# Causal scores on 64x64 tiles of TensorE: 24 instructions of 64 columns for 16 of 128, with two head pairs' keys exchanged

## What is computed

```python
def _attn_ref(r, k, v, w, u):            # 2 batches, 8 heads, 768 steps, 48 channels
    state = 0
    for t in range(S):
        y[:, :, t] = r_t @ (state + (u * k_t) v_t^T)
        state = w_t[:, None] * state + k_t v_t^T
x = y by token                           # 1536 x 384
g = elu(x @ w_in); x = g @ w_out         # 384 -> 2048 -> 384
p = domain_probs / sum
out = sum over 4 experts e of p[:, e] * (relu(x @ w1[e]) @ w2[e])
```

## Time and profile before

| what | us |
|---|---|
| median of 3 runs | 646.91 (646.85 to 646.93) |
| profiled execution, its own time | 646.69 |
| its span in the profile | 644.9 |
| TensorE busy in the span | 638.4 |
| VectorE busy | 418.6 |
| GpSimd busy | 296.0 |
| ScalarE busy | 237.1 |

### The profile page before, as it was taken

How to read it: one execution, slowest core, us unless ns; L and a number is a source line. 1 busy time by engine, 2 the same in 40 slices (tenths; PEclk the granted TensorE clock), 3 DMA queues, 4 the chain that set the end, 5 groups by cost and what they waited for, 6 DMA issues and landing times.

```text
span 644.9 us, 13796 instructions
## 1 busy us (share of the span) xinstructions
PE 638.4 (99%) x5046; PEld 591.5 (92%) x5046; DVE 418.6 (65%) x786; ACT 237.1 (37%) x557; POOL 296.0 (46%) x370
## 2 busy tenths in 40 slices
PE   8999999999999999999999999999999999999998
PEld 5998999877788888999999999999999999999997
DVE  7889999865357666565655555565656565656564
ACT  4785555655455554222222222222222222222221
POOL 5897424420499999996029900029900018000000
PEclk9999999999999999999999999999999999999999
DMA  8954454300000233000012100013100011001011
GB/s 322 403 193 137 138 183 164 124 11 1 1 2 1 73 98 99 27 1 1 1 50 99 50 1 0 1 49 99 50 1 0 0 50 50 0 1 49 0 50 50
DMA packets 19043, 42.34 MB, mean 66 GB/s; under 512 B 2608, under 2 KB 8752, under 8 KB 18992
## 3 DMA queue, kind: packets, MB, share of 16 engines
q1 hardware_dynamic: 18704, 41.23, 18.6%
q10 hardware_dynamic: 288, 0.39, 0.2%
HBM read 37.16 MB, written 4.46 MB: 65 GB/s over the span
## 4 chain that ended last, share of the span: by engine, by line
PE 90%; DVE 4%; POOL 3%; issue 1%; DMA 0%; ACT 0%; DVEq 0%; POOLq 0%
PE bank L1365 29%; PE bank L1366 29%; PE bank L1367 29%; POOL w_lo L546 3%; PE bank L1199 1%; PE bank L1278 1%; DVE fr L863 1%; PE bank L1290 1%; DVE fr L882 1%; DVE att L921 0%; DMA rkw<-rkw_dram 0%; DVE w_lo L966 0%; DVE bank L996 0%; PE bank L1232 0%; PE bank L1298 0%
## 5 line engine op out<-in xcount | busy, mean ns | idle before, releaser
L1365 PE MATMUL bank<-x_lo,w_hi 128*128 128x256 f32 (+2 forms) x416 | 138.1, 332 | 0.5 <-POOL w_lo L546 0.3
L1366 PE MATMUL bank<-x_hi,w_lo 128*128 128x256 f32 (+2 forms) x416 | 135.2, 325 | 0.0
L1367 PE MATMUL bank<-x_hi,w_hi 128*128 128x256 f32 (+2 forms) x416 | 135.2, 325 | 0.0
L1366 PE MATMUL bank<-w_hi,g_lo 128*128 128x384 f32 x384 | 129.6, 338 | 0.0
L1367 PE MATMUL bank<-w_hi,g_hi 128*128 128x384 f32 x384 | 129.3, 337 | 0.0
L1365 PE MATMUL bank<-w_lo,g_hi 128*128 128x384 f32 x384 | 129.0, 336 | 0.0
L826 ACT ACTIVATE g_hi<-bank 128x512 fp32r<-128x512 f32 x96 | 57.5, 598 | 144.3 <-DVE bank L1052 122.4
L1365 PEld LDWEIGHTS bank<-x_lo,w_hi 128*128 128x128 f32 x416 | 78.2, 188 | 10.4 <-issue 2.5
L1367 PEld LDWEIGHTS bank<-x_hi,w_hi 128*128 128x128 f32 x416 | 78.3, 188 | 7.4
L1366 PEld LDWEIGHTS bank<-x_hi,w_lo 128*128 128x128 f32 x416 | 78.3, 188 | 7.1
L1045 DVE TENSOR_TENSOR u_sum<-p_copy,bank 128x256 f32<-128x256 f32 x56 | 23.6, 421 | 92.1 <-ACT p_copy L750 91.3
(11 more groups left out here) (134 smaller groups left out, 1258.8 us busy)
## 6 DMA issues: line engine op xcount, KB each, us to landing
raw<-w_dram SPq DMA_DIRECT2D x48, 384.0 KB, 3.7
rkw<-rkw_dram SPq DMA_DIRECT2D x10, 772.5 KB, 4.5
tok<-tok_dram SPq DMA_DIRECT2D x10, 576.0 KB, 5.9
k_blocks_dram<-k_blocks SPq DMA_DIRECT2D x8, 256.0 KB, 4.1
kt_sb<-k_blocks_dram SPq DMA_DIRECT2D x32, 64.0 KB, 2.0
out_dram<-acc SPq DMA_DIRECT2D x10, 192.0 KB, 1.9
rkw<-rkw_dram SPq DMA_DIRECT2D x2, 512.0 KB, 4.4
rkw<-rkw_dram SPq DMA_DIRECT2D x2, 260.5 KB, 3.3
```

The lines of the kernel that those rows point to most:

```text
L1365: pe.matmul(out, wh, ml, start=start, stop=False, skip_group_check=shared)
L1366: pe.matmul(out, wl, mh, start=False, stop=False, skip_group_check=shared)
L1367: return pe.matmul(out, wh, mh, start=False, stop=stop, skip_group_check=shared)
```

## The change

Scores of the chunks 2 to 11 are no longer made for the block that is masked altogether (second half of the keys, first half of the queries). The three others are made one by one, 64 keys by 64 queries: 24 instructions of 64 columns in place of 16 of 128. So that each of the four tiles gets six of them, the first two pairs have the halves of their keys exchanged in `att` (partitions 0 to 63 hold the second half of the keys), and a pair with exchanged keys and one without stand side by side in `att` (`place`).

What follows from it: the rows of `tok` must be exchanged for the first four heads, which takes three transfers in place of one, with rows of three pieces of 192 numbers; the turned keys must be exchanged, which takes three transposes in place of one; the diagonal is set in three instructions for two; both copies wait for all three; the mask is there twice, once exchanged, by two more small transfers at the start.

```diff
+        def exchanged(p):
+            return p < PAIRS // 2
+        def place(c, p):
+            return p if c < FIRST else p % 2 * 2 + p // 2
...
         def diagonal_done(c):
-            return 2 * (c + 1 - FIRST)
+            return 3 * (c + 1 - FIRST)
...
-                sp.dma_start(tok[c % DEEP][:, :], tok_d[c]).then_inc(s_tok[c % DEEP], 16)
+                def columns(t, first):
+                    return t.rearrange("p (s n) -> p s n", s=3)[:, :, first:first + DM // 2]
+                here, there = tok[c % DEEP], tok_d[c]
+                sp.dma_start(columns(here[0:HALF, :], 0), columns(there[HALF:CH, :], 0)).then_inc(s_tok[c % DEEP], 16)
+                sp.dma_start(columns(here[HALF:CH, :], 0), columns(there[0:HALF, :], 0)).then_inc(s_tok[c % DEEP], 16)
+                sp.dma_start(columns(here[:, :], DM // 2), columns(there, DM // 2)).then_inc(s_tok[c % DEEP], 16)
...
+            for rows, others in ((slice(0, HALF), slice(HALF, CH)), (slice(HALF, CH), slice(0, HALF))):
+                sp.dma_start(const[rows, 0:P], const_d[others, C_MASK:C_MASK + P]).then_inc(s_exchanged, 16)
...
+                diagonal(0, 0, HALF, HALF)
+                diagonal(0, HALF, HALF, 0)
+                diagonal(1, 0, CH, 0)
...
-                dve.transpose(k_blocks[:, :, :].rearrange("q t (a j) -> q t a j", a=PAIRS),
-                              raw_k(c).rearrange("q (a t i) -> q t a i", a=PAIRS, i=STRIP)).then_inc(s_kb, 1)
+                dve.transpose(turned[:, 0:2, 0:2, :], strips[:, 2:4, 0:2, :]).then_inc(s_kb, 1)
+                dve.transpose(turned[:, 2:4, 0:2, :], strips[:, 0:2, 0:2, :]).then_inc(s_kb, 1)
+                dve.transpose(turned[:, :, 2:4, :], strips[:, :, 2:4, :]).then_inc(s_kb, 1)
...
-                    dve.wait_ge(s_diag, diagonal_done(c) - 1 + o)
-                    dve.copy_predicated(att[:, o, :, :], masks.bitcast(I32), found).then_inc(s_att, 1)
+                    dve.wait_ge(s_diag, diagonal_done(c))
+                    found = banks["x"][o][:, :].rearrange("p (a t) -> p a t", a=PAIRS // 2)
+                    dve.copy_predicated(att[:, o, :, :].rearrange("p (a b) t -> p a (b t)", b=2),
+                                        both_masks.unsqueeze(1).broadcast_to([P, PAIRS // 2, 2 * CH]).bitcast(I32),
+                                        found).then_inc(s_att, 1)
...
-                        for half in range(2):
-                            keys = slice(p * CH + HALF * half, p * CH + HALF * half + HALF)
-                            ins = pe.matmul(banks["x"][o][HALF * half:HALF * half + HALF, cols], k[rows, keys],
-                                            q[rows, cols], start=True, stop=True)
+                def block(p, o, later, first, count):
+                    rows, at = slice(64 * o, 64 * o + D), HALF * (later != exchanged(p))
+                    out = place(c, p) * CH + first
+                    return pe.matmul(banks["x"][o][at:at + HALF, out:out + count],
+                                     k[rows, p * CH + HALF * later:p * CH + HALF * later + HALF],
+                                     q[rows, p * CH + first:p * CH + first + count], start=True, stop=True)
+                for p in range(PAIRS // 2):
+                    for one in (p, p + PAIRS // 2):
+                        for later in range(2):
+                            for o in range(2):
+                                block(one, o, later, HALF, HALF)
+                    for one in (p, p + PAIRS // 2):
+                        for o in range(2):
+                            ins = block(one, o, 0, 0, HALF)
```

More of the change, by code:

```diff
@@ L294, in bass_linear_attention_elu_ffn_dense_experts, with tok_landed @@
         s_dr = sem("s_dr")
-        mask = const[:, C_MASK:C_MASK + P]
-        ident = const[:, C_ID:C_ID + P]
+        both_masks = const[:, 0:2 * P]
+        mask = const[:, P:2 * P]
+        ident = const[:, 2 * P:3 * P]
         def landed(eng, sems, c):
             eng.wait_ge(sems[c % DEEP], 16 * (c // DEEP + 1))
+        def tok_landed(eng, c):
+            parts = 3 * (c // DEEP + 1) - (2 if c % DEEP < FIRST else 0)
+            eng.wait_ge(s_tok[c % DEEP], 16 * parts)
+        def exchanged(p):
+            return p < PAIRS // 2
+        def place(c, p):
+            return p if c < FIRST else p % 2 * 2 + p // 2
         def raw_q(c):
@@ L532, in bonus_diagonal, with diagonal @@
                 pool.wait_ge(s_py, c)
[L533 to L537, removed]
+                heads = bonus_sb[:, c % 2, :]
+                found = att[:, :, :, :].rearrange("p o a t -> p (o a) t")
+                def diagonal(b, first, count, base):
+                    values = heads[:, b * PAIRS:(b + 1) * PAIRS].unsqueeze(2).broadcast_to([P, PAIRS, count])
+                    pool.affine_select(found[:, b:H:2, first:first + count], values, pattern=[[0, PAIRS], [1, count]],
+                                       compare_op=ALU.is_equal, fill=0.0, base=base, channel_multiplier=-1).then_inc(s_diag, 1)
+                diagonal(0, 0, HALF, HALF)
+                diagonal(0, HALF, HALF, 0)
+                diagonal(1, 0, CH, 0)
             def lo_w(n, half):
@@ L699, in copy_odd @@
             def copy_odd(c):
[L700 removed]
+                tok_landed(act, c)
                 need(act, s_py, c - 1)
@@ L910, in mask_scores @@
                     dve.wait_ge(s_px, c + 1)
+                    if c == FIRST:
+                        dve.wait_ge(s_exchanged, 32)
                     if c < FIRST:
@@ L1189, in scores @@
                 q, k = q_of(c), k_of(c)
[L1190 to L1194, removed]
-                            ins = pe.matmul(banks["x"][o][:, cols], k[rows, cols], q[rows, cols], start=True, stop=True)
-                            continue
-                        for half in range(2):
-                            keys = slice(p * CH + HALF * half, p * CH + HALF * half + HALF)
-                            ins = pe.matmul(banks["x"][o][HALF * half:HALF * half + HALF, cols], k[rows, keys],
-                                            q[rows, cols], start=True, stop=True)
+                if c < FIRST:
+                    for p in range(PAIRS):
+                        cols = slice(p * CH, (p + 1) * CH)
+                        for o in range(2):
+                            rows = slice(64 * o, 64 * o + D)
+                            ins = pe.matmul(banks["x"][o][:, cols], k[rows, cols], q[rows, cols], start=True, stop=True)
+                    ins.then_inc(s_px, 1)
+                    return
+                def block(p, o, later, first, count):
[10 more added lines that the diff above has]
+                    for one in (p, p + PAIRS // 2):
+                        for o in range(2):
+                            ins = block(one, o, 0, 0, HALF)
                 ins.then_inc(s_px, 1)
@@ L1289, in values_even @@
                     columns = STRIP // 2 if b % 3 == 1 else STRIP
-                    pe.matmul(strip_of(yt, b)[0:columns], v[:, first:first + columns], att[:, 0, p, :],
+                    pe.matmul(strip_of(yt, b)[0:columns], v[:, first:first + columns], att[:, 0, place(c, p), :],
                               start=False, stop=True, skip_group_check=True)
             def odd_strip(c, yt, b):
-                return pe.matmul(strip_of(yt, b), v_of(c)[:, b * STRIP:(b + 1) * STRIP], att[:, 1, b // 3, :],
+                return pe.matmul(strip_of(yt, b), v_of(c)[:, b * STRIP:(b + 1) * STRIP], att[:, 1, place(c, b // 3), :],
                                  start=False, stop=True, skip_group_check=True)
             def odd_end(c, yt, b):
-                return pe.matmul(strip_of(yt, b), v_odd[:, c % 2, b // 3, :], att[:, 1, b // 3, :],
+                return pe.matmul(strip_of(yt, b), v_odd[:, c % 2, b // 3, :], att[:, 1, place(c, b // 3), :],
                                  start=False, stop=True, skip_group_check=True)
```

28 lines of the change are left out of this document (16 added, 12 removed).

## The result

The changed kernel takes 649.57 us (median, 649.25 to 650.77), the kernel before 646.92 beside it. The ratio is 1.0045, 95% interval 1.0034 to 1.0055. The change costs 2.65 us, and the measured time lies above the range of the prediction.

What follows compares the result with a forecast made beforehand. TensorE, busy 638.4 of 644.9 us, was taken as the bound, with VectorE pacing chunks 5 to 7. Scores and VectorE gave -0.64, the keys' stall +0.2, about -0.4: 646.5 us, no change; range 645.3 to 648.3.

Steps and rivals of the forecast that it cites:

- Covered work: Diagonal's third instruction hidden by 1.8 us of cover; mask and longer tok transfers at the start costed at nothing.
- The turned keys: Keys' way through memory: tok 0.3 us longer (0 to 0.45), keys 0.6 later, TensorE 0.13 later.
- A stall of about 0.2 us in chunk 6, none elsewhere: TensorE's update waiting for the turned keys: 0.2 us in chunk 6 only, added to the sum.
- the 0.3 us that the prediction had named as a sign that it was wrong: Prediction wrong if an update row stands over 0.3 us behind the row ahead of it.
- rival 3: Turned keys come too late behind tok's short rows; update waits in chunks 3 to 7: 648.8 us, chance 0.13.
- The scores' gain of 0.17 us a chunk: TensorE's score group: 0.70 us for 0.87, 12 turns at 0.058; 1.7 us over ten chunks if TensorE never waits.
- Rival 4: Score MATMULs of 64 columns keep 0.0268 us start to start: 0.43 more a chunk, 651 us, chance 0.06.
- The transposes' 0.13 each: VectorE's three transposes take 0.755 us for 0.63: 0.13 more for each of chunks 2 to 9; bounds zero and 0.36.
- GpSimd's third instruction: Third instruction for the diagonal: some 0.1 us more, hidden by 1.8 us of cover before the copies.
- VectorE sets the pace around chunks 5 to 7: Between chunks 5 and 7 VectorE, at 0.13 us more a chunk, paces TensorE's scores for three chunks.
- The walk: Chunk-by-chunk lateness of TensorE against VectorE's scaled queries: chunk 7's scores 0.21 us late, 0.04 after them.
- chunks 8 to 11 keep all: VectorE has room from chunk 8 on, so four chunks keep 0.17 us each: 0.04 - 4 x 0.17 = -0.64.

Runs made afterwards that it cites:

- a_tok_host: Changed kernel with tok laid out exchanged in memory, so one transfer with rows of 4608 B again; mask transfers stay: 647.22 us, ratio 1.0005.
- b_tok_short: Kernel before with only tok cut into three transfers with rows of 768 bytes, nothing exchanged: 650.90 us, ratio 1.0068.
- a_host_turn_one: a_both_host with one transposition in place of three, leaving out the exchange of the keys that the update reads: 646.69 us, ratio 0.9998 to the kernel before.
- a_both_host: Changed kernel with tok exchanged in memory and both masks in the first transfer of constants: 647.42 us, ratio 1.0007 to the kernel before.
- a_slices_first: Changed kernel with weight slices 10 to 15 issued ahead of chunk 3's tok and the masks: 649.74 us, ratio 1.0042 to the kernel before.

## Why the prediction was wrong

**The step that failed** is the end of *Covered work*: "The two mask transfers and the longer `tok` transfers at the start lie in queues that are filled with weights used later. I cost them at nothing." The weights are used later, but not late enough. The DMA engines have no idle time from 16 to 32 us (a share of 1.02 and more in every window), so work put in makes all behind it late by its full length, and ScalarE reached for the first of the slices 10 to 15 while it was still in the queue. So the term for `tok` at the start, put at nothing, is 1.3 us of queue time for each of two transfers, and the short rows in all cost 2.4 us of the kernel's time. The masks cost about nothing, as was said. a_tok_host and b_tok_short show it from both sides.

**A size that was off**, in *The turned keys*: 0.3 us more for each `tok`, with 0.45 as the upper bound. By the packets above each `tok` took 1.3 us more. I had taken the price per KB from other transfers, with rows of 512 bytes, in a window with the DMA engines a third busy, so the bound was no bound. The load explains only a part: after 40 us, where the queues are emptier, `tok`'s packets still take 51 ns in the mean.

For short rows the Trainium skill (DMA: Bandwidth & Descriptors, section Why small descriptors are slow (HBM only)) gives a fixed 3 cycles a packet beside one for each 32 bytes. By that a row of 768 bytes takes 27 cycles for 24, an eighth more, and one of 4608 bytes 147 for 144: as an estimate 0.2 us on `tok`'s 1.7. The traces disagree: a mixture with such rows lost 19% of the rate (1303 for 1618), and a `tok` transfer took 1.3 us more. The measurement decides.

**The rest of the chain.** "A stall of about 0.2 us in chunk 6, none elsewhere": chunk 6's update did not wait, those of chunks 2, 4 and 5 did, two of them by more than the 0.3 us that the prediction had named as a sign that it was wrong. So rival 3 named the right mechanism (keys that come late behind `tok`), which I gave 0.13; its place, the chunks 3 to 7, was right for the smaller part only. The larger part hit at and before chunk 2, first through the weight slices, which no rival named. The prediction knew the queues to be filled there and put no price on it. That rival 3's 648.8 us lies near the measured time is in part luck.

**What held.** The scores' gain of 0.17 us a chunk: 0.86 for 1.03, with 12 turns of 0.058. Rival 4, a floor of 0.0268 for each MATMUL, is out: it would have shown a row of 1.4, and the row is 0.93. The turns are read from single starts: 107 ns for the first, 58 to 59 for the others. The transposes' 0.13 each: 0.75 for 0.63. GpSimd's third instruction, put at some 0.1 and covered: chunk 6's diagonal takes 1.37 us for 1.22. That VectorE sets the pace around chunks 5 to 7 as soon as the scores are shorter: a_host_turn_one.

**What was off beyond `tok`.** With the transfers undone (a_both_host) 647.4 us stand against the 646.5 of the forecast, so the `tok` step alone does not make the forecast right. The walk had chunk 7's scores 0.21 late; in a_both_host they begin at 97.99, 0.83 late, with chunk 5's late keys (0.4, below) among it. From there on "chunks 8 to 11 keep all" was to give 0.68 by the scores of chunk 11 (those of chunks 7 to 10) and gave 0.16: they begin at 157.40, against 156.73 before. a_both_host's waits name the reason:

```profile
PEld bank L1406 <- DVE x_lo L1034: 0.9, 2, 0.7
...
PEld bank L1406 <- DVE x_lo L1039: 0.4, 1, 0.4
```

One of the two waits for L1034 lies at 118.8 us, where the next tile of x begins: VectorE has room on the average of a slice there, but not at the step that TensorE waits for. In the kernel before, TensorE's operand load has no such wait between 110 and 125 us.

## What to carry to other kernels

A queue that is busy without a gap gives no cover by itself: price added transfer work at its full length, for whatever lies behind it, and look how much slack the first user of that has. Read the price of a row's length in a loaded window, and prefer to rearrange data in memory once over cutting a transfer into short rows. A gain on the busiest engine arrives only in those stretches where no other engine sets the pace, so count these stretches before counting instructions.

## What I had not expected of the hardware

- Rows of 768 bytes cost a fifth of the whole queue rate where they were 1.2 of 5.2 MB (326, 341, 294, 342 GB/s for 408, 406, 400, 404), rows of 1536 bytes 2% (394, 401, 386, 404).
- A DMA issue takes SP 0.33 us when the queues are free, 0.55 to 0.61 with short rows and 1.5 to 2.2 in the stretch where they are full (3.12 for two masks, 2.15 for a write in a_slices_first). So a full queue also seems to hold back SP's own program.
- Single issues of SP last about 1 us longer than their kind, at a place that moves from kernel to kernel: a_both_host's four loads of chunk 5's keys

```profile
76.11 2.82 SPq L472 DMA_DIRECT2D kt_sb<-k_blocks_dram  x4
```

take 2.82 us where the kernel before has

```profile
75.34 1.75 SPq L459 DMA_DIRECT2D kt_sb<-k_blocks_dram  x4
```

and the update that waits for them is 0.4 us later for it. In a_host_turn_one the same four take 2.64, end 0.3 us earlier, and the update has no wait. The kernel before has one too, at chunk 6 (2.54). I did not try what causes them.
